# Expert weights waited for one expert at a time, expert 5 loaded earlier, and batch 3's routing steps moved one tile later

## The reference

```python
def _moe2_ref(x, w_gate, w_local, w1, w2):
    B, S, D = x.shape                      # 4, 768, 320
    logits = np.einsum('bsd,de->bse', x, w_gate)          # 8 experts
    local_gate = 1.0 / (1.0 + np.exp(-np.einsum('bsd,de->bse', x, w_local).squeeze(-1)))
    for b in range(B):
        prev_e = -1
        for s in range(S):
            fresh_e = int(np.argmax(logits[b, s]))
            if s == 0 or local_gate[b, s] < 0.5:
                e = fresh_e
            else:
                e = prev_e if prev_e >= 0 else fresh_e
            prev_e = e
            ...                            # p = softmax of the logits
            h = np.maximum(x[b, s] @ w1[e], 0.0)          # 320 -> 1024
            out[b, s] = p[e] * (h @ w2[e])                # 1024 -> 320
```

## Time and profile before

| | us |
|---|---|
| median of 3 runs | 1028.56 |
| lowest and highest of them | 1028.43 to 1030.43 |
| the profiled execution | 1028.26 |
| its span, first to last instruction | 1026.5 |

### The profile page before, as it was taken

One profiled execution on the slowest core, in us unless ns is written; L12 is line 12 of the kernel. 1 busy time (PEld: TensorE's weight loads), 2 busy tenths in 40 slices (PEclk: granted clock), 3 DMA queues, 4 the chain that ended last, 5 costly groups with the idle time before them and its releaser, 6 DMA issues.

```text
span 1026.5 us, 51860 instructions
## 1 busy us (share of the span) xinstructions
PE 974.2 (95%) x23581; PEld 772.9 (75%) x23582; DVE 482.2 (47%) x998; ACT 262.7 (26%) x441; POOL 269.9 (26%) x297
## 2 busy tenths in 40 slices
PE   4689999999999999999999999996999999999996
PEld 3678898999989995556556556565888888888884
DVE  6457888778887742332232232252442322323230
ACT  1134444444444442102102112111111111111110
POOL 4436555665556620000020020020341010101101
PEclk9789999999999999999999999999999999999998
DMA  5225343323334223910110110049121111001000
GB/s 142 62 93 192 112 122 98 118 91 105 112 100 122 83 58 102 341 40 1 39 39 1 39 39 1 0 154 321 65 75 33 38 32 32 22 27 32 26 28 3
DMA packets 56903, 80.58 MB, mean 78 GB/s; under 512 B 22114, under 2 KB 36910, under 8 KB 56848
## 3 DMA queue, kind: packets, MB, share of 16 engines
q1 hardware_dynamic: 32816, 58.08, 18.1%
q10 hardware_dynamic: 21008, 13.06, 4.9%
q0 software_dynamic: 3024, 8.72, 2.4%
HBM read 66.99 MB, written 14.45 MB: 79 GB/s over the span
## 4 chain that ended last, share of the span: by engine, by line
PE 93%; issue 3%; DMA 2%; POOL 1%; ACTq 1%; DVE 1%; ACT 0%; SPq 0%; POOLq 0%; DVEq 0%
PE ps_D L1435 13%; PE ps_D L197 12%; PE ps_G L1424 8%; PE ps_E L1424 8%; PE ps_B L207 5%; PE ps_E L924 5%; PE ps_G L178 3%; PE ps_E L178 3%; PE ps_G L186 3%; PE ps_E L186 3%; PE ps_D L1007 3%; PE ps_E L922 3%; PE ps_A L898 2%; PE ps_D L958 2%; PE ps_D L898 2%
## 5 line engine op out<-in xcount | busy, mean ns | idle before, releaser
L1435 PE MATMUL ps_D<-room,hT 128*128 x496 | 138.7, 433 | 0.8 <-issue 0.8
L197 PE MATMUL ps_D<-room 128*128 128x384 f32 x384 | 126.3, 488 | 0.6 <-DVE room L262 0.6
L1435 PEld LDWEIGHTS ps_D<-room,hT 128*128 128x128 f32 x496 | 91.8, 190 | 35.7 <-issue 1.3
L197 PEld LDWEIGHTS ps_D<-room 128*128 128x128 f32 x384 | 72.4, 190 | 50.3 <-DVE room L262 1.3
L1388 POOL DMA_INDIRECT out<-y,token x31 | 30.5, 983 | 291.3 <-DVE y L1541 291.3
L1424 PEld LDWEIGHTS ps_G<-xTt,w_own 128*128 128x128 f32 x744 | 89.4, 195 | 13.7 <-issue 6.5
L518 POOL DMA_INDIRECT sorted_rows<-rows,slot x24 | 23.8, 991 | 286.3 <-DVE slot L510 280.2
L1424 PE MATMUL ps_G<-xTt,w_own 128*128 128x128 f32 x744 | 90.0, 278 | 8.9 <-issue 6.4
L862 POOL TENSOR_TENSOR room<-room 32x256 f32<-32x256 f32 x96 | 69.4, 723 | 105.7 <-DVE room L1278 100.3
L1524 DVE COPY w_own<-room 128x1024 f32 x62 | 43.2, 698 | 114.0 <-PE ps_G L1424 59.9
L1424 PE MATMUL ps_E<-xTt,w_own 128*128 128x128 f32 x744 | 88.1, 275 | 0.0
(11 more groups left out here) (211 smaller groups left out, 1524.6 us busy)
## 6 DMA issues: line engine op xcount, KB each, us to landing
room<-in_moe_w SPq DMA_DIRECT2D x8, 1280.0 KB, 13.5
room<-in_moe_w SPq DMA_DIRECT2D x8, 1024.0 KB, 11.1
room<-in_kb SPq DMA_DIRECT2D x48, 160.0 KB
room<-in_vt SPq DMA_DIRECT2D x24, 320.0 KB, 3.0
x_in<-sorted_rows ACTq DMA_DIRECT2D x27, 161.0 KB, 2.2
room<-in_w SPq DMA_DIRECT2D x48, 82.7 KB
room<-in_a SPq DMA_DIRECT2D x48, 80.0 KB
room<-in_r SPq DMA_DIRECT2D x48, 80.0 KB
```

The source lines that it names most:

```text
L197: mm = pe.matmul(self.vs_bank[n % 2][:, 0:TH], self.v[:, s, d * P:(d + 1) * P], self.wspT[:, s, t * TH:(t + 1) * TH], start=(s == 0), stop ...
L1435: mm = pe.matmul(self.ps_y, side.hT[:, u % 2, f, :], self.weights.w2[:, bass.ds(e, 1), f, :], start=(f == 0), stop=(f == self.NF - 1))
```

## The change

The memory: `wspT` moves up to begin with slot 6, so that slot 5 holds only `xT` and `win` (in part).

The weights: each expert gets a semaphore of its own, and POOL, at the start of its list for the experts, waits for them in the order 0 to 7 and adds one to a further semaphore, `ready`, after each. A tile of expert e waits for `ready` of e + 1.

SP: expert 5 is loaded as soon as the last group of hidden values of batch 3 is made (`h_made`), ahead of the waits for the first table and of the fetches of tiles 0 to 3. Then come 4 and 6 together, and 7. The wait for the early four is gone there.

The steps of batch 3's routing: on ACT `turned_x` of tile 1 goes ahead of `copy_rows` and `split_rows`; `copy_expert` and `copy_counts` come a tile later. On PE `turn_back` and `count` come a tile later, on DVE `weigh`, `place` and `other_tiles`, on POOL `scatter` and the blank rows. `split_rows`, `scan` and `join_rows` keep their tile.

```diff
@@ Gated
-        self.xT, self.win, self.wspT = sb("xT", NK, SEQ), sb("win", NK, D_FF), sb("wspT", TILES, SEQ)
+        self.xT, self.win = sb("xT", NK, SEQ), sb("win", NK, D_FF)
+        sb = Carver(room, (EARLY + 2) * EXPERT_FLOATS, (EXPERTS - 1) * EXPERT_FLOATS)
+        self.wspT = sb("wspT", TILES, SEQ)
@@ ExpertWeights
-        self.loaded = ctx.enter_context(nc.semaphore("experts_loaded"))
+        self.loaded = [ctx.enter_context(nc.semaphore(f"expert{e}_loaded")) for e in range(EXPERTS)]
+        self.ready = ctx.enter_context(nc.semaphore("experts_ready"))
@@
-            eng.dma_start(dst, src).then_inc(self.loaded, 16)
-
-    def until_early(self, eng):
-        eng.wait_ge(self.loaded, 16 * self.PARTS * EARLY)
+            eng.dma_start(dst, src).then_inc(self.loaded[e], 16)
+
+    def enter(self, eng, e):
+        eng.wait_ge(self.loaded[e], 16 * self.PARTS)
+        eng.sem_inc(self.ready, 1)
@@ until_loaded
-        eng.wait_ge(self.loaded, (e // EARLY) * (16 * self.PARTS * EARLY) + 16 * self.PARTS * EARLY)
+        eng.wait_ge(self.ready, e + 1)
@@ Experts.sync
+        sp.wait_ge(gated.h_made, GROUPS2 * BATCH)
+        weights.load(sp, EARLY + 1)
         routing.until_first(sp)
         sp.wait_ge(routing.first_known, 1)
         for u in range(self.SLOTS):
             self.fetch(sp, 0, u)
-        weights.until_early(sp)
         sp.wait_ge(gated.gated, 2 * ND * BATCH)
-        for e in range(EARLY, EXPERTS - 1):
+        for e in (EARLY, EARLY + 2):
             weights.load(sp, e)
@@ Experts.gpsimd
-        self.peeled(pool, self.put, 0, 2)
+        for e in range(EXPERTS):
+            self.weights.enter(pool, e)
+        self.peeled(pool, self.put, 0, 3)
         routing.scatter(pool, self.LAST)
-        self.peeled(pool, self.put, 2, 3)
+        self.peeled(pool, self.put, 3, 4)
         routing.fill_blank_rows(pool, range(0, 4))
-        self.peeled(pool, self.put, 3, 4)
+        self.peeled(pool, self.put, 4, 5)
         routing.fill_blank_rows(pool, range(4, EXPERTS))
-        self.peeled(pool, self.put, 4, self.PEELED * self.SLOTS)
+        self.peeled(pool, self.put, 5, self.PEELED * self.SLOTS)
@@ Experts.tensor
-        self.peeled(pe, self.tile_pe, 0, 1)
+        self.peeled(pe, self.tile_pe, 0, 2)
         routing.turn_back(pe, self.LAST)
-        self.peeled(pe, self.tile_pe, 1, 2)
+        self.peeled(pe, self.tile_pe, 2, 3)
         routing.count(pe, self.LAST)
-        self.peeled(pe, self.tile_pe, 2, FIRST - 1)
+        self.peeled(pe, self.tile_pe, 3, FIRST - 1)
@@ Experts.scalar
         self.relu(act, 0, 0)
+        self.turned_x(act, 0, 1)
         routing.copy_rows(act, self.LAST)
         routing.split_rows(act, self.LAST)
-        self.turned_x(act, 0, 1)
         self.peeled(act, self.tile_act, 0, 1)
         routing.join_rows(act, self.LAST)
+        self.peeled(act, self.tile_act, 1, 2)
         routing.copy_expert(act, self.LAST)
-        self.peeled(act, self.tile_act, 1, 2)
+        act.wait_ge(routing.first_known, 1)
+        self.peeled(act, self.tile_act, 2, 3)
         routing.copy_counts(act, self.LAST)
-        act.wait_ge(routing.first_known, 1)
-        self.peeled(act, self.tile_act, 2, FIRST - 3)
+        self.peeled(act, self.tile_act, 3, FIRST - 3)
@@ Experts.vector
-        self.peeled(dve, self.tile_dve, 0, 1)
+        self.peeled(dve, self.tile_dve, 0, 2)
         routing.weigh(dve, self.LAST)
-        self.peeled(dve, self.tile_dve, 1, 2)
+        self.peeled(dve, self.tile_dve, 2, 3)
         routing.place(dve, self.LAST)
-        self.peeled(dve, self.tile_dve, 2, 3)
+        self.peeled(dve, self.tile_dve, 3, 4)
         routing.other_tiles(dve)
-        self.peeled(dve, self.tile_dve, 3, FIRST - 2)
+        self.peeled(dve, self.tile_dve, 4, FIRST - 2)
```

## The result

The changed kernel takes 1016.48 us (median of 5 runs, 1015.21 to 1018.08), the kernel before, run beside it, 1028.56. The ratio is 0.9882 with a 95% interval of 0.9867 to 0.9896: faster by 1.2%. The forecast was 1016.6.

The account below looks back on a forecast made before the run. PE was taken as the bound, 93% of the span; 1.78 (x), 1.68 (turn back), 6.40 (weights), 1.80 (clock) and some 0.3 of small gaps made 12.0 us: 1016.3 profiled, 1016.6 us forecast, range 1015.4 to 1020.0.

Parts of the forecast that it names:

- The sum: PE's tile starts: tile 1 at 699.73, tile 2 at 709.73, tile 4 at 730.3 instead of 742.32, 12.0 us won.
- The time to spare at tile 2: DVE's first half of tile 2's weights ready at 709.6, PE wants it at 709.7: 0.1 us to spare.
- The join's "at most 4.9 us": Batch 3's small DMA ahead of PE's turn back: out at 708.4, at most 4.9 us, while PE comes at 719.7.
- 1.78 for x: Tile 1's x copied ahead on ACT: hidden values of tile 1 at 699.73 instead of 701.51, 1.78 us won.
- 1.68 for the turn back: PE's wait before batch 3's turn back, 1.68 us, gone once that step stands a tile later.
- 6.40 and 1.80 for weights and clock: PE's wait before tile 2, 6.40 us, and 1.80 us for matmuls at the lower clock behind it, both won.
- A: 22%: small transfers decide; batch 2's join beside expert 5's load costs 0.9 us, batch 3's rows 1 us: 1018.5.
- B: 5%: wrong expert early; tile 2 needs expert 7, its copies start at 711.2, PE waits 2.6 us: 1019.2.
- C: 6%: another PE wait, long enough for the clock to fall, 3 to 4 us and 1.8 for the clock: 1022.
- D: 3%: slower; small row transfers wait 14.9 us like the weights, 24.2 us lost against 12.0 won: 1040.8.
- The relay on POOL: POOL reaches it at 678.1; cost under 2.4 us, within 3.7 us of slack, so 0 of the path.
- The doubt from the section "Latency and other measured facts": Memory latency rises from 0.2 to 2 us at high load, so batch 2's join could complete up to 1.8 us later.

Follow-up runs that it names:

- e10: Changed kernel with ACT's copy of batch 3's transposed row values done four times more, so rows and scan come later: 1017.32 us, stretch 72.66 against 72.03.
- e4: Kernel before with only ACT's copy of tile 1's x moved ahead of the row transfers: 1029.35 us, ratio 0.9996 to 1.0029.
- e7: Probe: kernel before with batch 2's turn back one group of matmuls earlier on PE, so PE shows the join's landing: single run 1031.13 us.
- e6: Changed kernel with batch 3's routing steps a tile sooner again, as before; tile 1's x stays ahead: 1017.67 us, ratio 0.9871 to 0.9943.
- e1: Changed kernel with expert 5 loaded in its old place, behind expert 4, own waits kept: 1016.75 us, ratio 0.9867 to 0.9900.
- e8: Probe: changed kernel with batch 2's turn back one group of matmuls earlier on PE, expert 5's load right behind the join: single run 1018.26 us.
- e2: Changed kernel, expert 5 still early, but tiles of expert 4 or above wait for all eight: 1023.14 us, ratio 0.9921 to 0.9964.
- e3: Changed kernel's weights (own waits, expert 5 early) with every list's order from the kernel before: 1019.67 us, ratio 0.9889 to 0.9922.
- e5: Changed kernel with only ACT's copy of tile 1's x back behind the row transfers: 1019.68 us, ratio 0.9888 to 0.9941.
- e12: Second profile of the e5 kernel, on another chip, one run: 1020.33 us, stretch 75.40 us.

## Why the prediction was right

**The sum.** All in before's time:

| step | predicted | measured |
|---|---|---|
| batch 2's turn back | 658.4 | 658.43 (by taking 0.93 off) |
| tile 1's hidden values | 699.73 | 699.65 |
| scan | 706.63 | 706.28 |
| tile 2's hidden values | 709.73 | 709.75 |
| tile 3's | 719.9 | 719.99 |
| tile 4's | 730.3 | 730.46 |

The gain of 11.86 us in the stretch against 12.0 is right step by step. That the medians agree as closely (1016.48 and 1016.6) is partly luck, since the runs spread over 2.9 us.

**What was mis-sized, without harm.** The time to spare at tile 2 is 0.5 us (e10), not 0.1. The rows were issued at 699.76 instead of 699.96, since ACT's small copies overlap, and they took 4.95 us instead of the 5.11 of before. The join's "at most 4.9 us" was a price from full traffic (4.85 and 4.72 in e4 and e7); in thin traffic it is 2.3 (e6), and with nothing beside it 1.1 (e7).

**What was right in sum and wrong in its parts.** The prediction split the 12.0 us by the waits of before: 1.78 for x, 1.68 for the turn back, 6.40 and 1.80 for weights and clock. As parts of the change they are worth something else. The weights, early load included, take 9.90, since PE's wait at the turn back is gone too, in thinner traffic; x ahead alone takes nothing (e4), and with the weights but not the later steps 0.70. The sum only held because all three came together.

**What the prediction didn't ask.** It worked out that tile 2 could start at 694.8, 13.6 us before DVE got to it at 708.4. Without the early load expert 5 would have been the second to land, at 689.3 + 13.2 = 702.5 by the landings of before (weight DMAs 7 and 8 of 16):

```profile
L292 SPq DMA_DIRECT2D room<-in_moe_w x2: 587/592/597, 688.6 to 689.3; - x2
...
DMA to landing us min/median/max: 10.5/11.8/13.2
```

That is still 5.9 us ahead of DVE. The subtraction, left out, says that for tile 2 the early load is idle; e1 showed it.

**The rivals.** A's first half is out (e7, e8), its second is real in kind (e10) but did not occur. B is out: tile 2 is released by the scan and not by a weight DMA, in e1 too with expert 5 second in line. C did not occur here; e2 shows its price, 3.04 us of wait and 1.75 for the clock. D is out with the 4.95 us. The relay on POOL held nobody on the path. The Trainium skill's rule, on its page "DMA: Bandwidth & Descriptors", section "Queues, rings and completion order", that on each DMA engine a queue is worked off in its order and the queues take turns, fits all of it: ACT's row transfers were there after 4.95 us, among weight transfers that took up to 14.6, and e8 shows no delay by the load behind in the same queue. e8 is no test of the order, since the two hardly overlapped. The doubt from the section "Latency and other measured facts" rests on a figure that the page gives for the latency of the HBM, the memory outside the cores, at high load. The prediction carried it over to a transfer between partitions, which has both its ends in the core's own memory. At batch 2's join nothing of it is met, since that transfer is over as the load's data begins to flow. The join does take longer in traffic, 4.92 us against 2.33 (e6), but no run shows whether a latency or the taking of turns makes it.

## What to carry to other kernels

A counter shared by several loads makes every user wait for the last one. Going back to it in the changed kernel cost 4.89 us (e2), and own semaphores together with the early load gave 9.90 of 11.86 us in the old order (e3). Loading the needed expert earlier added nothing to own semaphores in the new order (e1); in the old order that is not shown. Before working on an earlier load, subtract its landing from the time at which its first user could start anyway. Waits in a row on one engine are not a sum of independent prices: a step removed ahead of a later wait is given back there, so each part is to be priced with the others in place.

## What the runs showed of the hardware

- A 3 KB transfer between partitions took 1.12 us from the end of its issue to its user on quiet DMA engines (e7), 2.33 in thinning traffic (e6) and 4.92, 4.85 and 4.72 in full traffic (e4, e7).
- One expert's weights (2560 KB), queued right behind such a transfer in the same queue, did not delay it: e7 and e8 agree to 0.01 us. The load's data began to flow as the transfer landed (DMA share 0.02 from 655 to 656, 0.82 from 656 to 657), so two overlapping transfers of one queue are not covered by this.
- A gap of 2.53 or 2.54 us on PE was followed by matmuls at a granted clock of 0.74 and 0.69 in e5, by 24 matmuls that took 4.43 us instead of 2.94 in e12, and by full clock in three other profiles (the kernel before, e3, e7) with a gap of 2.52 or 2.53 us. For such a gap a forecast has to carry both cases, 1.5 (e12) to 1.7 us (e5) apart here. Behind the waits of 5.53 and 6.40 us before tile 2 it had fallen each time (e4), as behind e2's 3.04.
